# A small addition and a normalising step of VectorE read a second tensor instead of a constant or a second scalar

## The reference

```python
# 1. attention: 2 batches, 8 heads, 768 positions, head dimension 64
scores = scale * q @ k.T - slope * dist          # only a local window and 8 global keys are kept
a = exp(scores - max(scores))
a = a / (sum(a) + 1e-09)                         # the small addition
x = a @ v                                        # then laid out as (2, 768, 512)
# 2. token mixing, then channel mixing
u = x + (relu(x.T @ w_tok1) @ w_tok2).T
x = u + relu(u @ w_ch1) @ w_ch2
# 3. gated block: 512 columns of U and 512 of V
h = relu(x @ w_in);  u, v = h[..., :512], h[..., 512:]
v_n = (v - mean(v)) / sqrt(var(v) + 1e-06)       # the normalising of V tiles
v_s = w_spatial @ v_n + b_spatial
out = (u * v_s) @ w_out
```

## Time and profile before

| what | us |
|---|---|
| median of three runs | 475.12 |
| lowest and highest of them | 475.12, 477.65 |
| the profiled execution, whole time | 476.14 |
| its span, first to last instruction | 474.1 |
| its time around the span | 2.04 |
| its mean granted TensorE clock | 0.995 of full |

### The profile page before, as it was taken

The page is one execution under the profiler, slowest core; times in us unless marked ns, Lnnn a source line. Parts: engine busy times, 40 slices in busy tenths (PEclk is TensorE's granted clock), DMA queues, the critical chain, the costliest instruction groups (busy, mean ns, idle before and its releaser), DMA issues.

```text
span 474.1 us, 6965 instructions
## 1 busy us (share of the span) xinstructions
PE 465.6 (98%) x2620; PEld 395.1 (83%) x2620; DVE 186.5 (39%) x521; ACT 156.9 (33%) x415; POOL 129.7 (27%) x145
## 2 busy tenths in 40 slices
PE   7999999999999999999999999999989999999997
PEld 3777777899888888888888888888889898899985
DVE  7899988246322112411114211105762054214230
ACT  4988887257211111311112221114422114322112
POOL 5377764334122221400003122222760002300000
PEclk9999999999999999999999999999989999999999
DMA  8477673135211111000000010030000100100012
GB/s 319 176 278 285 229 279 128 29 108 178 68 66 44 46 44 46 0 1 0 0 1 0 2 44 22 1 109 15 0 1 0 68 0 1 56 12 1 1 43 90
DMA packets 13906, 33.10 MB, mean 70 GB/s; under 512 B 1584, under 2 KB 3248, under 8 KB 13872
## 3 DMA queue, kind: packets, MB, share of 16 engines
q1 hardware_dynamic: 13584, 31.86, 19.3%
q10 hardware_dynamic: 288, 0.79, 0.5%
HBM read 29.49 MB, written 3.15 MB: 69 GB/s over the span
## 4 chain that ended last, share of the span: by engine, by line
PE 92%; DVE 4%; ACT 2%; issue 1%; DMA 1%; ACTq 0%; DVEq 0%
PE ps L392 25%; PE ps L394 25%; PE ps L393 25%; PE ps L1085 6%; PE ps L1127 5%; PE ps L1099 4%; PE ps L1198 1%; DVE V L1043 1%; DVE stats L1034 1%; ACT V L703 1%; DMA n_words<-in_n_both 1%; DVE xsum L1007 0%; DVE wo_h L382 0%; ACT Vn_h L718 0%; ACT prob L612 0%
## 5 line engine op out<-in xcount | busy, mean ns | idle before, releaser
L1019 DVE SCALAR_TENSOR_TENSOR R_l<-ps,R_h 128x512 fp32r<-128x512 f32 x36 | 24.9, 692 | 134.9 <-ACT R_h L689 134.9
L689 ACT ACTIVATE R_h<-ps 128x512 fp32r<-128x512 f32 x36 | 21.4, 595 | 130.5 <-PE ps L394 130.5
L394 PE MATMUL ps<-UT_h,wc_l 128*128 128x512 f32 x144 | 56.0, 389 | 0.0
L393 PE MATMUL ps<-UT_l,wc_h 128*128 128x512 f32 x144 | 56.0, 389 | 0.0
L392 PE MATMUL ps<-UT_h,wc_h 128*128 128x512 f32 x144 | 56.0, 389 | 0.0
L612 ACT ACTIVATE prob<-prob,neg_max 128x256 f32<-128x256 f32 (+1 forms) x96 | 45.8, 480 | 4.8 <-DVE neg_max L851 4.6
L577 POOL TENSOR_TENSOR UT_l<-xsum,UT_h 128x512 fp32r<-128x512 f32 x12 | 16.2, 1363 | 84.3 <-ACT UT_h L680 84.3
L392 PE MATMUL ps<-R_h,wc2a 128*128 128x512 f32 x96 | 37.3, 389 | 0.0
L393 PE MATMUL ps<-R_l,wc2a 128*128 128x512 f32 x96 | 37.3, 389 | 0.0
L394 PE MATMUL ps<-R_h,wc2a 128*128 128x512 f32 x96 | 37.3, 389 | 0.0
L392 PE MATMUL ps<-wsp_h,Vn_h 128*128 128x384 f32 x96 | 32.9, 342 | 2.2 <-DVE xsum L1007 2.2
(11 more groups left out here) (134 smaller groups left out, 1002.6 us busy)
## 6 DMA issues: line engine op xcount, KB each, us to landing
vv<-in_v_pairs SPq DMA_DIRECT2D x8, 768.0 KB, 4.4
kk<-in_k_pairs SPq DMA_DIRECT2D x7, 768.0 KB, 7.9
staged<-in_moe_w_ch SPq DMA_DIRECT2D x20, 256.0 KB, 2.9
out<-out_sb SPq DMA_DIRECT2D x12, 256.0 KB, 2.0
qT<-in_q_pairs SPq DMA_DIRECT2D x7, 384.0 KB, 6.4
staged<-in_moe_w_spatial SPq DMA_DIRECT2D x9, 256.0 KB, 2.6
staged<-in_moe_w_in SPq DMA_DIRECT2D x8, 256.0 KB, 2.5
staged<-in_moe_w_tok SPq DMA_DIRECT2D x6, 256.0 KB, 4.8
```

The costliest lines, as they stand in the source:

```text
L393: pe.matmul(o, a[0], b[1], start=False, stop=False, skip_group_check=True)
L394: return pe.matmul(o, a[1], b[0], start=False, stop=stop, skip_group_check=True)
L689: act.activation(R[0][:, f % 3, :], ps[:, 4 + f % 4, :], ACT.Relu).then_inc(ring_hi, 1)
L1019: dve.scalar_tensor_tensor(out=R[1][:, f % 3, :], in0=ps[:, 4 + f % 4, :], scalar=0.0, in1=R[0][:, f % 3, :].bitcast(F32), op0=ALU.max, op ...
```

## The change

Three edits, all on DVE.

- A new tile `eps` of 128x1 in SBUF is filled with 1e-09 at the start; DVE waits for that fill.
- `add_eps` adds `eps`, read with step 0 for all four sums of a row, by a tensor_tensor in place of a tensor_scalar with an immediate constant. The operands are given as 128x4 instead of 128x2x2.
- `v_tile` normalises by a scalar_tensor_tensor: the mean stays a scalar of each row; the inverse deviation, which was a second scalar, is read as a second tensor of 128x512 with step 0.

```diff
@@ tiles
+        eps = fixed("eps", [P, 1], F32)
@@ start of DVE
             dve.memset(oT[:, :, :], 1.0).then_inc(ones_ready, 1)
+            step(dve.memset(eps[:, :], 1e-09))
             dve.wait_ge(pool_setup, 3)
@@ add_eps
                 dve.wait_ge(probs_ready, 4 * (j + 1))
-                dve.tensor_scalar(recip[:, j % 2, :, :], sums[:, j % SUMS, :, :], 1e-09, None, ALU.add).then_inc(den_ready, 1)
+                dve.tensor_tensor(recip[:, j % 2, :, :].rearrange("p a b -> p (a b)"),
+                                  sums[:, j % SUMS, :, :].rearrange("p a b -> p (a b)"),
+                                  eps[:, 0:1].broadcast_to([P, 2 * BATCH]), ALU.add).then_inc(den_ready, 1)
@@ v_tile
                     dve.wait_ge(ln_recip, m + 1)
-                    dve.tensor_scalar(V32[:, m % 3, :], V32[:, m % 3, :], mean_var[:, old, 0:1], std[:, old, 2:3],
-                                      ALU.subtract, ALU.mult).then_inc(vv_norm, 1)
+                    dve.scalar_tensor_tensor(out=V32[:, m % 3, :], in0=V32[:, m % 3, :], scalar=mean_var[:, old, 0:1],
+                                             in1=std[:, old, 2:3].broadcast_to([P, FG]), op0=ALU.subtract,
+                                             op1=ALU.mult).then_inc(vv_norm, 1)
```

## The result

Over 19 runs each, interleaved, the changed kernel takes 478.09 us at the median (477.35 to 481.25) and the kernel before 475.62 (474.69 to 477.65). The ratio is 1.0056 with a 95% interval of 1.0042 to 1.0070: 2.5 us slower by the medians, well clear of noise, and inside 1%. (2.5 is the difference of the medians; by the ratio it is 2.7.) The forecast was 477.0, its range 475.0 to 479.2. The profiled execution took 478.70 us with a span of 476.9, 2.8 us more than the 474.1 of before.

The account below looks back on a forecast made before the run. TensorE bounds the kernel, except where the first batch's normalisings lie on the chain: 0.17 + 1.08 + 0.19 = +1.4 us. That gives 477.6 from the profiled 476.14, or 476.5 by the median; forecast 477.0, range 475.0 to 479.2.

Parts of the forecast that it names:

- What bounds the kernel, and where the change can act: TensorE is busy 98% of the span; only the first batch's V tiles, 323 to 345 us, leave it and decide.
- The small addition waits for POOL in either form: 24 additions in attention: both forms wait where POOL reads SBUF, median stays near 692 ns, cost about 0.
- The undisturbed normalising: First batch, two tiles: 0.69 us instead of 0.52 and 0.55, giving +0.17 and about +0.19 on the chain.
- The disturbed ones, +0.27 each: First batch, four tiles: DVE ends 0.55 us behind POOL's end instead of 0.28; delays add up to 1.08.
- Rival A: Step-0 tensor doesn't wait for POOL: each normalising 0.69 us, wait shrinks to 0.6, total 472.9 us; chance 0.07.
- Rival C: scalar_tensor_tensor with step-0 tensor takes twice the time, 1.38 us: +4.1 on the chain, total 481.7 us; chance 0.04.
- The wait of TensorE: Before s_part: its wait for line 1007 of part x2 grows from 2.2 to about 3.6 us in total.
- The clock: Behind TensorE's wait: one slow stretch losing 1.6 us again, so no change; bounds none (-1.6) and a second (+1.6).
- rival B: The longer wait of TensorE costs a second slow clock stretch, +1.6 us: total 479.2 us; chance 0.13.
- The total: Whole kernel: 477.6 us from the profiled execution, 476.5 by the median of three runs; 477.0 taken, halfway.
- The second batch: Six normalisings, +0.17 us each, covered by DVE's idle time and Vn wanted two parts later: cost 0.

Follow-up runs that it names:

- eps_only: Kernel before with only the new small addition and the fill of eps, normalising as before; 476.02 us, ratio 0.9997 to before.
- norm_second: Kernel before with the new normalising in the second batch alone; 476.21 us, ratio 1.0007 to before.
- norm_first: Kernel before with the new normalising in the first batch alone (6 of 12); 479.17 us, ratio 1.0057 to before.
- after_best: Changed kernel, POOL's four wo_l splits moved directly behind its first batch's last Vn_l, DVE's last wo_h behind part x2; 474.06 us, ratio 0.9962 to kernel before.
- kernels with the matmuls: Unused matmuls fill TensorE's wait ahead of s_part: 12 in the kernel before (475.06 us, ratio 0.9982), 18 in the changed one (476.32 us, 1.0013).
- norm_only: Kernel before with only the new normalising, in both batches, small addition as before; 478.08 us, ratio 1.0051 to before.
- before_pool6: Kernel before with POOL's four wo_l splits moved directly behind its last Vn_l of the first batch; 474.50 us, ratio 0.9969 to before.
- after_pool6: Changed kernel with POOL's four wo_l splits moved directly behind its last Vn_l of the first batch; 475.68 us, ratio 0.9983 to kernel before.
- before_best: Kernel before, POOL's four wo_l splits moved directly behind its first batch's last Vn_l, DVE's last wo_h behind part x2; 473.23 us, ratio 0.9945 to before.

## Why the prediction was right, and where it was off

- *What bounds the kernel, and where the change can act*: right. Only the stretch from 323 to 345 us matters; eps_only and norm_second show the rest to be free, norm_first shows the stretch to carry all.
- *The small addition waits for POOL in either form*: right, median 686 ns for 692, and attention is as it was. The form loses nothing at this size: the shortest take 152 ns for 158. The Trainium skill, SBUF — State Buffer, section "Who interferes with whom", says that a DVE instruction with two SBUF inputs contends with a GpSimd instruction that reads SBUF, just as one in a two-port mode does; this case's traces agree, with 1.51 us beside POOL for 0.52 alone in the old form and 1.82 for 0.72 in the new.
- *The undisturbed normalising*: 0.72 us for the forecast 0.69 against 0.52, and 0.75 for the last of the first batch.
- *The disturbed ones, +0.27 each, adding up*: right. 1.21, 0.94, 1.82 and 1.82 us for 0.96, 0.68, 1.55 and 1.51; the six sum to 7.26, forecast 7.2. Line 1007 moved by 1.54, forecast 1.4.
- *Rival A*, a step-0 tensor escapes POOL: out, since the longest is 1.82. *Rival C*, twice the time: out, since the least is 0.72.
- *The wait of TensorE*: forecast 3.6 in total, measured 3.7. But "TensorE waits for DVE only once" was true of the list of waits and not of the kernel: the wait of block u0 for part x0 was there, about 0.1 us long, and became 0.3. It doesn't add to the total while the later wait absorbs it; in after_best it does.
- *The clock*: this is the term that was mis-sized. "I take one such stretch again", so a change of 0. That took the one profiled execution of before for all of them. In 41 of 98 timed ones the kernel before has no slow stretch to lose; with the longer wait all 40 have one or more. On the mean that is 1.2 to 1.3 us (1.0 to 1.2 by the kernels with the matmuls). Forecast +1.4 and measured +2.5 differ by this. The profiled execution of the changed kernel has 6.2 us of slow clock in place of 3.2, which is rival B to the letter, but those of norm_only and norm_first have 3.2 behind the same wait: what the typical execution adds is a first slow stretch where there was none, and a second one only in some.
- *The total*: 477.0 is 1.1 below the median measured, and the range holds 478.09 since it was drawn to take in B. The base of 475.6, halfway between two values, is what 19 runs gave (475.62); three runs couldn't tell that, so it was luck. With this base right, the 1.1 is the clock.
- *The second batch*: the cost of 0 was right. DVE's idle time, one of its two covers, was misread (2.89 us a tile instead of 2.72, as said). That a later normalising meets POOL's Vn_l for 0.4 us more didn't come: in norm_second all take 0.72 or 0.75.

## What to carry to other kernels

In this kernel the form that reads a second tensor was slower at 128x512 in SBUF (0.72 us for 0.52), even though that tensor is one value a row read again and again; at 128x4 nothing of it shows. It gained nothing against POOL: both forms wait for POOL's instruction. Whether the step-0 tensor or the operation scalar_tensor_tensor as such costs the 0.2 us wasn't separated; every one of 128x512 on record reads two tensors.

Look beside a DVE instruction of unexpected length for the POOL instruction that ends just before it does. Taking POOL's splits out of the way was worth 1.5 us here, and 2.6 to 2.8 with the DVE split moved too, about as much as the change of form cost. But list first who waits for the work that is moved.

And when a delay lengthens an idle time of TensorE, price the clock behind it, too, over many executions: here that was 1.0 to 1.3 us, nearly as much as the delay's own 1.3 to 1.6.

## What the runs showed of the hardware

- A DVE instruction with one SBUF tensor and two scalars of a row (128x512, 0.52 us alone) ends 0.28 us behind the POOL instruction that holds it up; the one with two SBUF tensors (0.72 alone) ends 0.55 behind. So 0.24 and 0.17 us of the time that each takes alone are spent during the wait. That this is the fixed part of the instruction and the rest the streaming of the 512 elements fits the two to one, but no run here tests it.
- A second tensor with step 0 is read about as slowly as a full one: 0.72 us here, 0.69 for line 1010's undisturbed instructions of two full tensors (another operation, tensor_tensor).
- The granted clock behind the same wait of 3.4 us isn't the same in each execution. It was low for 6.2 us in the profiled one of the changed kernel, for 3.2 us in norm_only's (348.0 to 351.2), and for 3.2 us in norm_first's:

```profile
348.30:351.50 3.20, 3.20 (x10) 3.20 (x11) 2.45 (x3) 1.64 (x3) 3.20 (x3) 0.50 0.00 0
```

  A single profile can't price such a wait. Behind the waits of 1.2 us in before_pool6 and 1.6 us in after_pool6 the profiled clock stayed at full rate (1.00 from 346 to 354 us in both).
- All of norm_first's first batch lies 1.6 us later than the changed kernel's, although until then the two differ only in the small addition. The windows show it as clock again: attention, 10 to 90 us, had a mean granted clock of 0.98, with TensorE busy for 79.8 us, and 1.00 in the kernels before and after. 80 x 0.02 are the 1.6 us. They lie in one stretch: from 10.8 to 13.8 us the clock was 0.50, behind TensorE's wait of 1.2 us in attention. after_best's and after_pool6's show 0.98 as well; before_best's and before_pool6's don't, so these pairs are compared by their timed runs and not by their spans. Some executions are that much later before they come to the place of the change. norm_first's row:

```profile
10.00:90.00 80.00, 79.83 (x773) 61.50 (x772) 67.97 (x280) 63.14 (x234) 49.22 (x72) 0.98 0.59 214
```
